# Expert rows in transposable stripes: VectorE in place of TensorE for turning the token rows

## The chip, the cores and the metric

One core of a Trainium2 chip runs the whole program. The metric is the device time of one execution in microseconds. TensorE (PE) multiplies, VectorE (DVE) and ScalarE (ACT) work elementwise, GpSimd (POOL) issues the indirect transfers, and SyncE (SP) issues the plain ones, in the order of its program: while it waits for a semaphore, nothing behind that wait is issued.

## The reference, cut to what matters

The input is 4 sequences of 3072 tokens with 256 features. A two-dimensional Fourier transform is taken (real part), each token then goes to one of 8 experts, and a channel mix follows.

```python
X = np.fft.fft(np.fft.fft(x, axis=1), axis=2).real
# expert stage, N = 12288 tokens, D = 256, F = 1024, 8 experts
expert_idx = np.argmax(logits, axis=1)
for e in range(E):
    mask = expert_idx == e
    h = np.maximum(x[mask] @ w1[e], 0.0)
    out[mask] = gate_w[mask, None] * (h @ w2[e])
# channel mix on out: two mixes with the previous token, relu^2, sigmoid
```

## The kernel before

The program has three stages. The Fourier stage (to about 209 us of the span) works through four batches; it leaves each batch's spectrum in `xr` (24 slots of 128 tokens), and GpSimd scatters these rows, sorted by expert, into the DRAM tensor `rows`. A row there is 256 features, the gate and the number of the row where the result belongs (`ROW` = 258 words, 1032 bytes). The expert stage (209 to 869 us) goes over `NB` = 55 blocks of `BT` = 256 rows, one block a step, each block of one expert only. The channel mix follows.

One step i of the expert stage, `m_step(i, s)` on each engine, with the buffer number s = i % 2:

- PE: `up` (48 matmuls of the first product, into four PSUM banks), `rows_in(i + 1)` (the next block's rows, four 128x128 transposes into PSUM bank 6), `down` (48 matmuls of the second product, in two halves j of 128 tokens).
- ACT: `hidden_a` four times (relu of a bank, the high part of `ht`), between them `w_high_part` (the next block's weights, high parts), `rows_a` (the high part of the next block's rows, `xgt`, from PSUM bank 6), and two `result` (gate times result, into `yo`).
- DVE: `hidden_v` four times (low part of `ht`), between them `w_low_part`, then `meta` (gates and row numbers out of `xg` into `gates` and `ids`), `rows_v` (low part of `xgt`), and two more `w_low_part`. In steps 0 to 5 it also finishes the gates and the block tables of the last batch.
- POOL: after each step's result, `scatter`: two indirect transfers of `yo` to the DRAM tensor `moe`, by `ids`. Ahead of the first of these stands the rest of the scatter of batch 2, in steps 4 to 7 stand six transfers each of batch 3, and in steps 12 to 14 one `w_split` subtraction each for the channel mix.
- SP: in `m_step(i)` it waits until block i's weights are split (`w_low`), issues `load_w(i + 2)` (2 MB, 128 pieces of 16 KB), waits for `m_meta` of step i (the buffer `xg[s]` is free then) and issues `load_rows(i + 2)` (one transfer of 258 KB, 128 pieces of 2064 bytes). Ahead of step 9 stand eight transfers of the padding rows (`load_tails`), ahead of step 10 three loads of the channel mix's weights. Each `load_w` and `load_rows` first reads its expert or its row number from SBUF (`value_load`).

All orders are written out by hand; every engine runs in program order. PE's `down(i)` waits for the four `hidden_v` of step i one after the other, its `up(i + 1)` for `rows_v`.

Of the kernel before, what the change touches and what calls it, by code (L numbers as in the profile page):

```python
# [28 lines left out]
P = 128  # L29
B, S, D = 4, 3072, 256  # L30
N2 = 24
J = 4
G = P // J
KP = N2 * J
NK = N2 // 2 + 1
# [42 lines left out]

C_ORDER = [0, 128] + list(range(2, 128, 2)) + list(range(1, 128, 2))
ORDER = C_ORDER + [D - c for c in C_ORDER[2:]]  # L80


def constants():
# [49 lines left out]
def fft_moe_channel_mix(nc, x, emb, tau, w_e, mu_k, mu_r, w_k, w_v, w_r, tab, out, rows, moe):  # L133
    ctx = ExitStack()
    with ctx:
        def sb(name, shape, dt=F32):
            return ctx.enter_context(nc.sbuf_tensor(name, shape, dt))[:]

        def sem(name):
            return ctx.enter_context(nc.semaphore(name))  # L140
# [43 lines left out]
        gates = [sb(f"gates{i}", [P, HB]) for i in range(2)]  # L184
        ids = [sb(f"ids{i}", [P, HB], I32) for i in range(2)]


        base = -(-nc.sbuf_base // 32) * 32
# [39 lines left out]
        yo_at = at[0]  # L228
# [14 lines left out]
        ht = part("ht", [2, FC, BT], F32R)  # L243
        assert at[0] <= xg_at
        at[0] = xg_at
        xg = [part(f"xg{n}", [HB, ROW]) for n in range(2)]
# [75 lines left out]
        m_meta = sem("m_meta")  # L322
        s_pad = sem("s_pad")
        s_half = sem("s_half")
        gathered = [sem(f"gathered{n}") for n in range(2)]
        m_xtr = sem("m_xtr")
        m_xt = sem("m_xt")
        m_up = sem("m_up")
        m_xh = sem("m_xh")
# [73 lines left out]
        def _(sp):  # L403
# [10 lines left out]
            def load_rows(i, s):  # L414

                r = sp.value_load(row_of[0:1, bass.ds(i, 1)], min_val=0, max_val=E * CAPR)
                sp.dma_start(xg[s].rearrange("p j c -> p (j c)"),
                             rows[bass.ds(r, BT), :].rearrange("(p j) c -> p (j c)", j=HB)).then_inc(gathered[s], 16)

            sp.dma_start(f1[:], tab["c_f1"]).then_inc(s_tab, 16)  # L420
            sp.dma_start(emb_in[0:E, :], emb).then_inc(s_emb, 16)
# [49 lines left out]
            def m_step(i, s):  # L471
                if i + 2 < NB:
                    sp.wait_ge(w_low, (i + 1) * WP)
                    load_w(i + 2, s)
                    sp.wait_ge(m_meta, i + 1)
                    load_rows(i + 2, s)

            for i in range(NB):
# [48 lines left out]
        def _(pe):  # L527
# [42 lines left out]
                    ins = mm(o, a(i), b_(k), start=first_ and n == 0, stop=last_ and n == 2)  # L570
                return ins

            def rows_in(i, s):
                pe.wait_ge(gathered[s], 16 * (i // 2 + 1))
                wait(pe, m_xt, i)
                for c in range(DC):
                    for j in range(HB):
                        last = tp(ps[:, 6, c * BT + j * P:c * BT + (j + 1) * P], xg[s][:, j, c * P:(c + 1) * P], ident[:])  # L578
                last.then_inc(m_xtr, 1)

            for b in range(B):

                for c in range(NC):
# [50 lines left out]
                for st in range(NK + 1):  # L634
                    if st < NK:
                        feature_dft(st)
                    if 0 <= st - 1 < NK:
                        sequence_dft(st - 1)
                    if b == B - 1 and st == NK - 2:
                        rows_in(0, 0)  # L640


            for n in range(2):
# [29 lines left out]

            def m_step(i, s):
                up(i, s)
                if not isinstance(i, int) or i + 1 < NB:
                    rows_in(i + 1, 1 - s)
# [76 lines left out]
        def _(act):  # L754
# [16 lines left out]
                copy(tot.rearrange("p h c -> p (h c)"), ps[0:TH * E, 7, 0:2 * P]).then_inc(d_totc, 1)  # L771

            def rows_a(i):
                act.wait_ge(m_xtr, i + 1)
                copy(xgt[:, 0, :, :].rearrange("p c t -> p (c t)"), ps[:, 6, :]).then_inc(m_xh, 1)

            def squares(b, k2):

# [49 lines left out]
            def result(i, s, j):  # L828
                act.wait_ge(m_down, i * HB + (j + 1))
                if j == 0:  # L830
                    act.wait_ge(m_meta, i + 1)
                    wait(act, scattered[s], i // 2 * (16 * HB))
                ins = nc.scalar.activation(yo[s][:, j, :], ps[:, 4 + j, 0:D], ACT.Copy,  # L833
                                           scale=gates[s][:, j:j + 1])
                ins.then_inc(m_y, 1)

            def m_step(i, s):
# [81 lines left out]
        def _(dve):  # L919
# [67 lines left out]
            def gate(b):  # L987
                link = chain(r_step, (b + 1) * R_STEPS + R_EXP)
                dve.wait_ge(r_exp, b + 1 + PRIME)
                link(v.tensor_reduce(gsum, ex, AX.X, ALU.add))  # L990
                link(v.tensor_scalar(gsum, gsum, 1e-9, None, ALU.add))
                link(v.reciprocal(gsum[:], gsum[:]))
                assert link.n[0] == R_STEPS - R_EXP
                xo = xr[XB[b]]
                copy(xo[:, 0:1, D:D + 1], gsum[:, 0:1].unsqueeze(2))
                copy(xo[:, 1:NK, D:D + 1], gsum[:, 1::2].unsqueeze(2))
                copy(xo[:, NK:N2, D:D + 1], gsum[:, N2 - 2:0:-2].unsqueeze(2))
                v.tensor_scalar(xo[:, :, D + 1:ROW], idc[:].unsqueeze(2), float(b * RB), None, ALU.add  # L998
                                ).then_inc(gate_done, 1)

            def place(b):
# [69 lines left out]
            def w_low_part(i, s, q):  # L1071
# [2 lines left out]
                v.tensor_tensor(we[s][:, 1, c0:c0 + WQ], we_raw[s][:, c0:c0 + WQ],  # L1074
                                we[s][:, 0, c0:c0 + WQ].bitcast(F32), ALU.subtract).then_inc(w_low, 1)

            def rows_v(i, s):
                dve.wait_ge(m_xh, i + 1)
                v.tensor_tensor(xgt[:, 1, :, :].rearrange("p c t -> p (c t)"), ps[:, 6, :],
                                xgt[:, 0, :, :].rearrange("p c t -> p (c t)").bitcast(F32), ALU.subtract).then_inc(m_xt, 1)  # L1080

            for b in range(B):
                xo = xr[XB[b]]
# [15 lines left out]
                for st in range(NK + 1):  # L1099
# [25 lines left out]
                        tier_b(False)  # L1125
                    if b == 2 and st == 10:
                        tier_c(False)
                    if b == B - 1 and st == NK - 1:
# [6 lines left out]
            def meta(i, s):  # L1135
                dve.wait_ge(gathered[s], 16 * (i // 2 + 1))
                wait(dve, m_y, i * HB - HB)
                wait(dve, scattered[s], i // 2 * (16 * HB))
                copy(gates[s][:], xg[s][:, :, D:D + 1].rearrange("p j o -> p (j o)"))
                copy(ids[s][:], xg[s][:, :, D + 1:ROW].rearrange("p j o -> p (j o)")).then_inc(m_meta, 1)  # L1140

            def hidden_v(i, n):
                dve.wait_ge(m_hh, i * (FC // 2) + (n + 1))
# [3 lines left out]

            def m_step(i, s):
                more = not isinstance(i, int) or i + 1 < NB
                hidden_v(i, 0)  # L1150
                if more:
                    w_low_part(i + 1, 1 - s, 0)
                hidden_v(i, 1)
                if more:
                    w_low_part(i + 1, 1 - s, 1)
                hidden_v(i, 2)
                hidden_v(i, 3)
                meta(i, s)
# [73 lines left out]
        def _(pool):  # L1232
# [10 lines left out]
            g.memset(tailc[:, :, D + 1:ROW], FAR).then_inc(d_init, 1)  # L1243
# [20 lines left out]
            moe_flat = moe.rearrange("b r c -> (b r) c")  # L1264

            def scatter(i, s):
                pool.wait_ge(m_meta, i + 1)
                for j in range(HB):
                    pool.wait_ge(m_y, i * HB + (j + 1))
                    g.indirect_dma_start(out=moe_flat, in_=yo[s][:, j, :], in_offset=None,  # L1270
                                         out_offset=bass.IndirectOffsetOnAxis(ap=ids[s][:, j:j + 1], axis=0),
                                         bounds_check=last_result, oob_is_err=False).then_inc(scattered[s], 16)

            for i in range(NB):
# [41 lines left out]
```

## Time and profile before

| what | us |
|---|---|
| runs, median of 3 (lowest, highest) | 1517.86 (1515.67, 1519.12) |
| the profiled execution | 1520.16 |
| its span, first to last instruction | 1518.4 |
| PE busy | 1470.5 (97%) |
| DVE busy | 1006.2 (66%) |
| ACT busy | 884.3 (58%) |
| POOL busy | 250.5 (17%) |
| mean granted TensorE clock | 0.986 |

The rows below come from the profile page and from queries of the same trace. Times are from the start of the span. In a timeline row, the bracket tells how long the engine had been idle and who released it. A busy share is a mean over stages; what a step costs is read from the chain that sets its end.

### The profile page before, as it was taken

Reading aid. Unit: us, or ns where it says so; the run is one execution under the profiler, and the core shown is the slowest. Engines: PE = TensorE matmul, PEld = TensorE weight load, DVE = VectorE, ACT = ScalarE, POOL = GpSimd, SP = SyncE. Lnnn points to the kernel's source line nnn. Section 1 sums busy time; section 2 is a strip of 40 time slices with the busy share of each in tenths; the row PEclk is TensorE's granted clock in tenths of the full one; section 3 lists DMA queues with packets and bytes.
Section 4 is the critical chain, followed back from the end, with each engine's and each line's share of the span. In section 5 each row is a group of like instructions: output and inputs, shape, how many; then the busy total and the mean of one; then the engine's idle time right before and its main releaser. Section 6 shows DMA issues by size and latency. Waiting matters only on the chain.

```text
span 1518.4 us, 29616 instructions
## 1 busy us (share of the span) xinstructions
PE 1470.5 (97%) x10894; PEld 1403.0 (92%) x10894; DVE 1006.2 (66%) x1765; ACT 884.3 (58%) x1706; POOL 250.5 (17%) x225
## 2 busy tenths in 40 slices
PE   6998889999999999999999879999999999999998
PEld 6887789999999999999999878999999998999998
DVE  4767776866666666666666456767576767667673
ACT  1654475666656666566665455656565656556563
POOL 2146436722311111111111100000000000000000
PEclk8999999999999999999999979999999999999999
DMA  8225366887656665666556111110111101010100
GB/s 245 67 76 156 107 215 236 292 291 275 216 214 233 224 213 208 212 230 231 211 208 214 64 42 56 29 55 28 52 31 32 51 28 55 28 55 28 55 14 28
DMA packets 64339, 201.47 MB, mean 133 GB/s; under 512 B 14246, under 2 KB 40725, under 8 KB 55576
## 3 DMA queue, kind: packets, MB, share of 16 engines
q1 hardware_dynamic: 54392, 175.42, 34.4%
q0 software_dynamic: 9888, 25.28, 4.5%
q8 instruction: 34, 0.56, 0.2%
q14 instruction: 25, 0.20, 0.0%
HBM read 160.44 MB, written 42.06 MB: 133 GB/s over the span
## 4 chain that ended last, share of the span: by engine, by line
PE 91%; DVE 3%; DMA 2%; ACT 1%; issue 1%; SPq 1%; POOL 1%; POOLq 0%; DVEq 0%; ACTq 0%
PE ps L570 78%; PE ps L596 4%; PE ps L630 3%; PE ps L697 1%; PE ps L578 1%; PE ps L619 1%; PE ps L620 1%; DMA we_raw<-w_e 1%; POOL rows L1252 1%; DVE we L1074 0%; SPq L486 0%; DMA tau_b<-tau 0%; DVE k2f L1209 0%; DMA moe<-yo,ids 0%; DVE k_split L1202 0%
## 5 line engine op out<-in xcount | busy, mean ns | idle before, releaser
L570 PE MATMUL ps<-we,ht 128*128 128x256 f32 x2640 | 330.5, 284 | 1.6 <-DVE ht L1144 1.6
L570 PE MATMUL ps<-xgt,we 128*128 128x256 f32 x2640 | 322.9, 282 | 4.6 <-DVE we L1074 3.8
L570 PEld LDWEIGHTS ps<-xgt,we 128*128 128x128 f32 x2640 | 317.5, 189 | 5.3 <-issue 4.2
L570 PEld LDWEIGHTS ps<-we,ht 128*128 128x128 f32 x2640 | 319.8, 188 | 2.5 <-DVE ht L1144 2.2
L570 PE MATMUL ps<-w_split,k_split 128*128 128x256 f32 x2304 | 280.5, 283 | 0.1
L570 PEld LDWEIGHTS ps<-w_split,k_split 128*128 128x128 f32 x2304 | 278.2, 192 | 0.3 <-DVE k_split L1202 0.3
L1074 DVE TENSOR_TENSOR we<-we_raw,we 128x1024 fp32r<-128x1024 f32 x220 | 263.3, 1217 | 16.7 <-ACT we L767 16.7
L1144 DVE SCALAR_TENSOR_TENSOR ht<-ps,ht 128x512 fp32r<-128x512 f32 x220 | 146.2, 684 | 192.3 <-ACT ht L825 192.2
L570 PE MATMUL ps<-x_split,w_split 128*128 128x512 f32 x1152 | 268.7, 393 | 4.4 <-DVE x_split L1196 4.4
L570 PEld LDWEIGHTS ps<-x_split,w_split 128*128 128x128 f32 x1152 | 216.7, 190 | 49.1 <-DVE x_split L1196 4.8
L897 ACT ACTIVATE relu<-ps 128x512 f32<-128x512 f32 x192 | 115.0, 599 | 205.2 <-PE ps L570 205.2
L767 ACT CAST we<-we_raw 128x1024 fp32r<-128x1024 f32 x220 | 226.0, 1055 | 3.5 <-DMA we_raw<-w_e 3.5
L825 ACT ACTIVATE ht<-ps 128x512 fp32r<-128x512 f32 x220 | 132.2, 602 | 99.0 <-PE ps L570 98.9
L1270 POOL DMA_INDIRECT moe<-yo,ids x110 | 111.3, 1012 | 448.5 <-ACT yo L833 443.1
L1209 DVE TENSOR_TENSOR k2f<-relu 128x512 f32<-128x512 f32 x192 | 132.9, 692 | 48.7 <-ACT relu L897 33.8
L833 ACT ACTIVATE yo<-ps,gates 128x256 f32<-128x256 f32 x110 | 52.1, 475 | 149.3 <-PE ps L570 144.4
L1202 DVE TENSOR_TENSOR k_split<-k2f,k_split 128x512 fp32r<-128x512 f32 x192 | 131.5, 685 | 2.1
L891 ACT CAST k_split<-k2f 128x512 fp32r<-128x512 f32 x192 | 117.8, 613 | 11.2 <-DVE k2f L1209 11.2
L1218 DVE TENSOR_TENSOR yc<-ps,sig 128x1024 f32<-128x1024 f32 x24 | 29.4, 1224 | 136.7 <-PE ps L570 136.7
L1252 POOL DMA_INDIRECT rows<-xr,pos x96 | 103.3, 1076 | 63.0 <-DVE xr L998 35.0
L1192 DVE SCALAR_TENSOR_TENSOR xmix<-xc,mu,tmix 128x512 f32<-128x512 f32 x96 | 67.9, 748 | 22.2 <-ACT tmix L879 22.2
L879 ACT ACTIVATE tmix<-xc,omm 128x512 f32<-128x512 f32 x96 | 64.2, 716 | 23.1 <-DVE xc L1186 20.2
(134 smaller groups left out, 1285.7 us busy)
## 6 DMA issues: line engine op xcount, KB each, us to landing
we_raw<-w_e SPq DMA_DIRECT2D x55, 2048.0 KB, 8.4
xg<-rows SPq DMA_DIRECT2D x55, 258.0 KB, 2.7
xin<-x SPq DMA_DIRECT2D x16, 768.0 KB, 5.8
xm<-moe SPq DMA_DIRECT2D x24, 512.0 KB, 3.9
out<-yc SPq DMA_DIRECT2D x24, 512.0 KB, 3.2
rows<-tailc SPq DMA_DIRECT2D x9, 258.0 KB, 2.9
moe<-yo,ids POOLq DMA_INDIRECT x110
f<-c_f SPq DMA_DIRECT2D x1, 1664.0 KB, 16.9
```

The lines of the kernel that those rows point to most:

```text
L570: ins = mm(o, a(i), b_(k), start=first_ and n == 0, stop=last_ and n == 2)
L767: copy(we[s][:, 0, c0:c0 + WQ], we_raw[s][:, c0:c0 + WQ]).then_inc(w_high, 1)
L825: nc.scalar.activation(ht[:, 0, 2 * n:2 * n + 2, :].rearrange("p f t -> p (f t)"), ps[:, n, :], ACT.Relu).then_inc(m_hh, 1)
L891: copy(k_split[:, 0, f, :], k2f[f % 2][:]).then_inc(c_kh, 1)
L897: nc.scalar.activation(relu[f % 2][:], ps[:, 2 + f % 2, :], ACT.Relu).then_inc(c_relu, 1)
L1074: v.tensor_tensor(we[s][:, 1, c0:c0 + WQ], we_raw[s][:, c0:c0 + WQ], we[s][:, 0, c0:c0 + WQ].bitcast(F32), ALU.subtract).then_inc(w_low, 1)
L1144: v.scalar_tensor_tensor(ht[:, 1, 2 * n:2 * n + 2, :].rearrange("p f t -> p (f t)"), ps[:, n, :], 0.0, ht[:, 0, 2 * n:2 * n + 2, :].rearra ...
L1192: v.scalar_tensor_tensor(xmix[:, m_, c, :], xc[s][:, c, 1:TC + 1], mu[:, m_, c:c + 1], tmix[:, m_, c, :], ALU.mult, ALU.add).then_inc(c_mi ...
L1202: v.tensor_tensor(k_split[:, 1, f, :], k2f[f % 2][:], k_split[:, 0, f, :].bitcast(F32), ALU.subtract).then_inc(c_kl, 1)
L1209: v.tensor_tensor(k2f[f % 2][:], relu[f % 2][:], relu[f % 2][:], ALU.mult).then_inc(c_k2, 1)
L1252: g.indirect_dma_start(out=rows, in_=xr[XB[b]][:, SLOTS[t], :], in_offset=None, out_offset=bass.IndirectOffsetOnAxis(ap=pos[:, b * N2 + t: ...
L1270: g.indirect_dma_start(out=moe_flat, in_=yo[s][:, j, :], in_offset=None, out_offset=bass.IndirectOffsetOnAxis(ap=ids[s][:, j:j + 1], axis= ...
```

## The change

The rows of a block no longer come as whole rows on 128 partitions, but as four stripes a = 0 to 3. Stripe a goes to partitions 32a to 32a + 31 and holds 64 features of all 256 tokens: partition 32a + i has, for each of 8 groups t of 32 tokens, features 64a to 64a + 63 of token 32t + i. In DRAM that is 256 pieces of 256 bytes a stripe, 1024 a block. One VectorE instruction (`rows_t`, 128x512) then transposes all 32x32 blocks into `xgf` in SBUF, which has the features on the partitions. TensorE's `rows_in` is gone. The order of the features on the partitions differs from before, so the first weight's rows are reordered on the host (`BLOCKS`). `rows_a` and `rows_v` read `xgf` and not PSUM.

Gate and row number come in a transfer of their own (`meta`, 256 pieces of 8 bytes), the row number as an integer, and ScalarE and GpSimd read them from there; VectorE's `meta` and its two small instructions are gone. The buffer `meta[s]` is free for block i only when the scatter of block i - 2 has landed, so SP waits for that scatter inside `load_rows`. The stripes' buffer is free as soon as `rows_t` has read it (`m_xf`).

```diff
             def load_rows(i, s):
                 r = sp.value_load(row_of[0:1, bass.ds(i, 1)], min_val=0, max_val=E * CAPR)
-                sp.dma_start(xg[s].rearrange("p j c -> p (j c)"),
-                             rows[bass.ds(r, BT), :].rearrange("(p j) c -> p (j c)", j=HB)).then_inc(gathered[s], 16)
+                for a in range(P // Q):
+                    sp.dma_start(xg[s][a * Q:(a + 1) * Q].rearrange("i t c f -> i t (c f)"),
+                                 rows[bass.ds(r, BT), a * DC * Q:(a + 1) * DC * Q].rearrange("(t i) f -> i t f", i=Q)
+                                 ).then_inc(gathered[s], 16)
+                if i >= 2:
+                    sp.wait_ge(scattered[s], (i - 2) // 2 * (16 * HB) + 16 * HB)
+                sp.dma_start(meta[s][:], rows[bass.ds(r, BT), D:ROW].rearrange("(j p) c -> p j c", j=HB)
+                             ).then_inc(meta_in[s], 16)
...
                     load_w(i + 2, s)
-                    sp.wait_ge(m_meta, i + 1)
+                    sp.wait_ge(m_xf, i + 1)
                     load_rows(i + 2, s)
...
-            def rows_in(i, s):
-                pe.wait_ge(gathered[s], 16 * (i // 2 + 1))
-                wait(pe, m_xt, i)
-                for c in range(DC):
-                    for j in range(HB):
-                        last = tp(ps[:, 6, c * BT + j * P:c * BT + (j + 1) * P], xg[s][:, j, c * P:(c + 1) * P], ident[:])
-                last.then_inc(m_xtr, 1)
...
             def rows_a(i):
-                act.wait_ge(m_xtr, i + 1)
-                copy(xgt[:, 0, :, :].rearrange("p c t -> p (c t)"), ps[:, 6, :]).then_inc(m_xh, 1)
+                act.wait_ge(m_xf, i + 1)
+                copy(xgt[:, 0, :, :], xgf[:]).then_inc(m_xh, 1)
...
+            def rows_t(i, s):
+                dve.wait_ge(gathered[s], 16 * (P // Q) * (i // 2 + 1))
+                wait(dve, m_xt, i)
+                v.transpose(xgf.rearrange("p c (t i) -> p c t i", i=Q), xg[s].rearrange("p t c f -> p c t f")
+                            ).then_inc(m_xf, 1)
...
             def m_step(i, s):
                 more = not isinstance(i, int) or i + 1 < NB
+                if more:
+                    rows_t(i + 1, 1 - s)
                 hidden_v(i, 0)
...
-                meta(i, s)
...
             def scatter(i, s):
-                pool.wait_ge(m_meta, i + 1)
+                pool.wait_ge(meta_in[s], 16 * (i // 2 + 1))
```

On SP the work around the loads of rows reads as follows in the program before; `we_raw_78` and `we_raw_79` are the two weight buffers, and this is the piece from the rows of block 2 to the weights of block 3:

```order
L416 TENSOR_LOAD row_of [waits m_meta]
L416 ISA x2
L417 ISA
L417 DMA xg_83<-rows 128x516
L411 TENSOR_LOAD expert_of [waits w_low]
L411 ISA x2
L412 ISA
L412 DMA we_raw_78<-w_e 128x4096
```

And the same place in the changed program, from the last stripe of block 2 to the first instruction for the rows of block 3:

```order
L421 DMA xg_83<-rows 32x8x64
L426 ISA [waits scattered0]
L426 DMA meta<-rows 128x2x2
L414 TENSOR_LOAD expert_of [waits w_low]
L414 ISA x2
L415 ISA
L415 DMA we_raw_78<-w_e 128x4096
L419 TENSOR_LOAD row_of [waits m_xf]
```

Between the rows of block 2 and the weights of block 3 there now stands a wait for the scatter of block 0 (`scattered0`); in general `load_w(i + 3)` stands behind the scatter of step i, which it did not before.

## Rows read from the trace of the kernel before

**Rows 1.** Chain of waits, 480 to 530 us: start, length, what.

```profile
483.69 0.44 PE ps L578 x4
484.13 11.43 PE ps L570 x96
```

**Rows 2.** Groups by line, VectorE: count, busy us, mean ns, idle before.

```profile
L1074 DVE TENSOR_TENSOR we<-we_raw,we 128x1024 fp32r<-128x1024 f32 x220 | 263.3, 1217 | 16.7 <-ACT we L767 16.7
...
L1202 DVE TENSOR_TENSOR k_split<-k2f,k_split 128x512 fp32r<-128x512 f32 x192 | 131.5, 685 | 2.1
```

**Rows 3.** Timeline of step 24, 501 to 514 us, all engines.

```profile
501.59 5.84 PE L570 MATMUL ps<-xgt,we 128*128 128x256 f32 x48
...
502.54 0.97 POOL L1270 DMA_INDIRECT moe<-yo,ids  x1 [1.28 <-ACT yo L833]
...
503.92 0.69 DVE L1144 SCALAR_TENSOR_TENSOR ht<-ps,ht 128x512 fp32r<-128x512 f32 x1 [3.76 <-ACT ht L825]
...
504.86 1.23 DVE L1074 TENSOR_TENSOR we<-we_raw,we 128x1024 fp32r<-128x1024 f32 x1 [0.25 <-ACT we L767]
...
507.74 1.28 DVE L1144 SCALAR_TENSOR_TENSOR ht<-ps,ht 128x512 fp32r<-128x512 f32 x2
...
509.67 2.35 DVE L1074 TENSOR_TENSOR we<-we_raw,we 128x1024 fp32r<-128x1024 f32 x2
...
512.76 0.33 SPq L412 DMA_DIRECT2D we_raw<-w_e  x1
```

**Rows 4.** Weight loads: the page's DMA issues, and the tile's time to landing.

```profile
we_raw<-w_e SPq DMA_DIRECT2D x55, 2048.0 KB, 8.4
...
DMA to landing us min/median/max: 7.7/8.4/12.5
```

**Rows 5.** DMA packets: 1019.2 to 1020.8 (1 KB), 1.75 to 2.05 (384 bytes), 871.4 to 871.8 us.

```profile
q1 hardware_dynamic: 477, 0.49, 100.5%
...
q1 hardware_dynamic: 94, 0.03, 48.9%
...
q0 software_dynamic: 48, 0.00, 7.7%
```

**Rows 6.** GpSimd's timeline, 223 to 248 us.

```profile
223.58 4.20 POOL L1260 TENSOR_TENSOR rinv<-sumsq,half 128x24 f32<-128x24 f32 x1 [21.12 <-ACT square L786]
...
245.09 0.97 POOL L1270 DMA_INDIRECT moe<-yo,ids  x1 [0.30 <-issue]
246.37 0.97 POOL L1270 DMA_INDIRECT moe<-yo,ids  x1 [0.30 <-issue]
```

**Rows 7.** Chain of waits, 200 to 400 us: start, length, what.

```profile
246.37 2.40 DMA moe<-yo,ids
...
249.84 5.94 PE ps L570 x48
...
337.53 12.53 DMA we_raw<-w_e
```

**Rows 8.** SP's timeline, 205 to 350 us: start, length of issue.

```profile
222.07 0.33 SPq L412 DMA_DIRECT2D we_raw<-w_e  x1
...
318.68 8.66 SPq L468 DMA_DIRECT2D rows<-tailc  x8
328.10 0.35 SPq L412 DMA_DIRECT2D we_raw<-w_e  x1
```

**Rows 9.** Timelines of PE (330 to 372 us) and of GpSimd (355 to 410 us).

```profile
333.09 5.84 PE L570 MATMUL ps<-xgt,we 128*128 128x256 f32 x48
...
359.19 5.84 PE L570 MATMUL ps<-xgt,we 128*128 128x256 f32 x48
...
371.05 1.11 PE L570 MATMUL ps<-xgt,we 128*128 128x256 f32 x8
...
374.45 1.86 POOL L1270 DMA_INDIRECT moe<-yo,ids  x1 [0.30 <-issue]
```

**Rows 10.** Busy time by windows; after the busy times the granted clock, DMA share, GB/s.

```profile
208.00:212.00 4.00, 2.40 (x11) 2.43 (x12) 3.72 (x4) 0.00 (x0) 0.00 (x0) 0.66 0.00 0
```

More of the change, by code:

```diff
@@ L32 @@
 J = 4
+Q = 32
 G = P // J
@@ L80 @@
 ORDER = C_ORDER + [D - c for c in C_ORDER[2:]]
+BLOCKS = np.arange(D).reshape(P // Q, D // P, Q).transpose(1, 0, 2).reshape(D)
 def constants():
@@ L183, in fft_moe_channel_mix @@
         row_of = sb("row_of", [1, NB], I32)
-        gates = [sb(f"gates{i}", [P, HB]) for i in range(2)]
-        ids = [sb(f"ids{i}", [P, HB], I32) for i in range(2)]
+        meta = [sb(f"meta{i}", [P, HB, 2]) for i in range(2)]
         base = -(-nc.sbuf_base // 32) * 32
@@ L227, in fft_moe_channel_mix @@
         emb_sq = part("emb_sq", [D])
-        yo_at = at[0]
+        yo_at = xg_at + 2 * HB * D + 3 * DC * BT
+        assert at[0] <= yo_at
         at[0] = yo_at + 2 * HB * D
@@ L245, in fft_moe_channel_mix @@
         at[0] = xg_at
-        xg = [part(f"xg{n}", [HB, ROW]) for n in range(2)]
+        xg = [part(f"xg{n}", [BT // Q, DC, Q]) for n in range(2)]
+        xgf = part("xgf", [DC, BT])
         xgt = part("xgt", [2, DC, BT], F32R)
@@ L321, in fft_moe_channel_mix @@
         w_in = [sem(f"w_in{n}") for n in range(2)]
-        m_meta = sem("m_meta")
         s_pad = sem("s_pad")
@@ L325, in fft_moe_channel_mix @@
         gathered = [sem(f"gathered{n}") for n in range(2)]
-        m_xtr = sem("m_xtr")
+        m_xf = sem("m_xf")
+        meta_in = [sem(f"meta_in{n}") for n in range(2)]
         m_xt = sem("m_xt")
@@ L638, in _ @@
                         sequence_dft(st - 1)
-                    if b == B - 1 and st == NK - 2:
-                        rows_in(0, 0)
             for n in range(2):
@@ L675, in m_step @@
                 up(i, s)
-                if not isinstance(i, int) or i + 1 < NB:
-                    rows_in(i + 1, 1 - s)
                 if isinstance(i, int) and i == 1:
@@ L830, in result @@
                 if j == 0:
-                    act.wait_ge(m_meta, i + 1)
+                    act.wait_ge(meta_in[s], 16 * (i // 2 + 1))
                     wait(act, scattered[s], i // 2 * (16 * HB))
                 ins = nc.scalar.activation(yo[s][:, j, :], ps[:, 4 + j, 0:D], ACT.Copy,
-                                           scale=gates[s][:, j:j + 1])
+                                           scale=meta[s][:, j, 0:1])
                 ins.then_inc(m_y, 1)
@@ L997, in gate @@
                 copy(xo[:, NK:N2, D:D + 1], gsum[:, N2 - 2:0:-2].unsqueeze(2))
-                v.tensor_scalar(xo[:, :, D + 1:ROW], idc[:].unsqueeze(2), float(b * RB), None, ALU.add
+                v.tensor_scalar(xo[:, :, D + 1:ROW].bitcast(I32), idc[:].unsqueeze(2), float(b * RB), None, ALU.add
                                 ).then_inc(gate_done, 1)
@@ L1075, in w_low_part @@
                                 we[s][:, 0, c0:c0 + WQ].bitcast(F32), ALU.subtract).then_inc(w_low, 1)
+            def rows_t(i, s):
[3 more added lines that the diff above has]
+                            ).then_inc(m_xf, 1)
             def rows_v(i, s):
                 dve.wait_ge(m_xh, i + 1)
-                v.tensor_tensor(xgt[:, 1, :, :].rearrange("p c t -> p (c t)"), ps[:, 6, :],
-                                xgt[:, 0, :, :].rearrange("p c t -> p (c t)").bitcast(F32), ALU.subtract).then_inc(m_xt, 1)
+                v.tensor_tensor(xgt[:, 1, :, :], xgf[:], xgt[:, 0, :, :].bitcast(F32), ALU.subtract).then_inc(m_xt, 1)
             for b in range(B):
@@ L1127, in _ @@
                         tier_c(False)
+                    if b == B - 1 and st == NK - 2:
+                        rows_t(0, 0)
                     if b == B - 1 and st == NK - 1:
@@ L1133, in _ @@
                 w_low_part(0, 0, q)
[L1135 to L1140, printed above, removed]
             def hidden_v(i, n):
@@ L1242, in _ @@
             pool.wait_ge(d_init, 1)
-            g.memset(tailc[:, :, D + 1:ROW], FAR).then_inc(d_init, 1)
+            g.memset(tailc[:, :, D + 1:ROW].bitcast(I32), int(FAR)).then_inc(d_init, 1)
             last_row, last_result = pool.to_reg(E * CAPR - 1), pool.to_reg(NROWS - 1)
@@ L1270, in scatter @@
                     g.indirect_dma_start(out=moe_flat, in_=yo[s][:, j, :], in_offset=None,
-                                         out_offset=bass.IndirectOffsetOnAxis(ap=ids[s][:, j:j + 1], axis=0),
+                                         out_offset=bass.IndirectOffsetOnAxis(ap=meta[s][:, j, 1:2].bitcast(I32), axis=0),
                                          bounds_check=last_result, oob_is_err=False).then_inc(scattered[s], 16)
@@ L1306 @@
         "w_e": c(np.concatenate([
-            moe_w1[:, ORDER, :].reshape(E, DC, P, F).transpose(0, 2, 1, 3).reshape(E, P, DC * F),
+            moe_w1[:, ORDER, :][:, BLOCKS, :].reshape(E, DC, P, F).transpose(0, 2, 1, 3).reshape(E, P, DC * F),
             moe_w2.reshape(E, FC, P, D).transpose(0, 2, 1, 3).reshape(E, P, FC * D)], 2)), "mu_k": c(moe2_mu_k.reshape(DC, P).T), "mu_r": c(moe2_mu_r.reshape(DC, P).T),
```

## The prediction, made before the changed kernel ran

> **What bounds the kernel now.** I read the chain of waits first. In the middle of the expert stage it is TensorE and nothing else: 11.43 us of products and 0.44 us of transposes in turn [rows 1], so a step of 11.87 us. The timeline of one step then tells how much room the others have. Counted from the start U of a step's `up` (501.59), VectorE begins its first low part at +2.33 after 3.76 us of idling, once more stands still for 0.25 us, and has its fourth low part done at 509.02, +7.43 [rows 3]. TensorE is ahead of nobody by much there, so what delays VectorE by more than about half a microsecond reaches TensorE. Last I read who issues the loads, and when. SP issues the weights of the block after next at 512.76, 0.74 us after the last low part of the weights (509.67 + 2.35) [rows 3]; that is 0.7 us before the next step begins. They land after 8.4 us in the median, 7.7 at the least [rows 4], against 13.9 us until ScalarE wants them. This lead of some 5.5 us is what the change spends.
>
> **What it removes.** The four transposes on TensorE, 0.44 us a step [rows 1]; there are 55 of them, 24.2 us, all on the chain. That is the whole gain there can be. VectorE's two small instructions went beside other work: nothing.
>
> **What it adds on VectorE.** One 128x512 instruction, `rows_t`. The trace has no such transpose. From below and as my value: the 512-column instruction out of SBUF, 0.69 us; from above, two passes, the 1024-column row, 1.22 us [rows 2]. It stands ahead of the first `hidden_v`, where VectorE idles for 3.76 us [rows 3]. As long as the stripes are there 0.7 us before +2.33 it costs nothing. If they come later, it holds all four low parts behind it. ScalarE's and VectorE's reads of `xgf` in place of PSUM: nothing, the wait is elsewhere.
>
> **What it adds in transfers.** 1024 pieces of 256 bytes for 128 of 2064. A piece's price: share times 16 engines times window by packets, so 1.005 x 16 x 1.6 / 477 = 54 ns for 1 KB, 0.489 x 16 x 0.3 / 94 = 25 ns for 384 bytes, and 0.077 x 16 x 0.4 / 48 = 10 ns for the smallest [rows 5]. 256 bytes lie between the last two, nearer to 25: I take 20 ns, 1024 x 20 / 16 = 1.3 us a block; the ends are 0.7 us and, should a piece cost as much as one of 1 KB, 3.5 us. The stripes are queued behind the weights, so this comes on top of the weights' landing. The Trainium skill, page "DMA: Bandwidth & Descriptors", first table, speaks against the change here: below 512 B a transfer is said to be done as read-modify-write. The 384-byte row does not show a jump (25 ns is under half of 54). By that rule, read as a doubled price, the stripes would take 2.6 us.
>
> **What it adds as a wait.** This is the dear part. SP now waits for the scatter of step i before it loads `meta` for block i + 2, and behind that wait are queued `load_w(i + 3)` and the stripes of block i + 3. In time from U of step i + 1, which is the end of step i: the second scatter is issued at 502.54, +0.95 [rows 3]; it lands 2.40 us later where no weight load is under way [rows 7]; `meta` is issued in some 0.4 us (0.33 for the instruction and a register or two); the expert's number is read and the weights issued 0.74 us on, together +4.5. In the kernel before this was -0.7. The weights land 8.0 us later (between 7.7 and 8.4, since one of two scatters no longer meets them), the stripes 1.3 us behind: +13.8 after the end of step i. They are wanted at the head of step i + 2, two steps on. From there to the end of that step: `rows_t` 0.69, from the first low part's start to the fourth one's end 5.10 less 0.25 of idling = 4.85 [rows 3], then 30 of the 96 products are left, 30 x 11.43 / 96 = 3.57, and 0.1 for the signal, together 9.2 us. So two steps together last at least 13.8 + 9.2 = 23.0, a step 11.5 us. TensorE alone would need 11.43. **I take 11.55** for the ordinary step: a gain of 0.32 and not of 0.44 us.
>
> **Where the hold is longer.** (a) *Step 2.* GpSimd is far behind here: after a `rinv` that waits 21.12 us for ScalarE (223.58) it has the rest of batch 2 to scatter, and the two scatters of step 0 are issued only at 245.09 and 246.37 [rows 6]. Nothing in the change makes this earlier. The second lands at 248.77 [rows 7]. Before, the weights of block 3 were issued at 222.07 [rows 8]; now at 248.77 + 0.4 + 0.74 = 249.9. They land at 258.2 (8.0, and 0.3 for the scatters of step 1 beside them), the stripes at 259.5. In step 2 ScalarE stands before `w_high_part(3)` and VectorE before `rows_t(3)`, and TensorE's `down(2)` gets no input from about 240 on. Its end is 259.5 + 9.2 = 268.7. The clock comes on top: where TensorE had idled ahead of the expert stage, the granted clock of 208 to 212 us was 0.66, so part of that stretch at 1.2 instead of 2.4 GHz [rows 10]; I add 1.5 us. Step 3 starts at 270.2 and not at 249.84 [rows 7]: **+20.4**. (b) *Steps 3 to 9*, with the rows of batch 3 on the DMA engines: weights 8.4 and 0.3 more give 11.85 a step, 83.0 against 333.09 - 249.84 = 83.25: **-0.3**. (c) *Steps 10 and 11.* The eight tails take SP 9.4 us (318.68 less 0.7 for reading the row number, to 327.34) [rows 8], and these now begin only after the scatter of step 8 and its `meta`, 0.95 + 2.40 + 0.4 = 3.75 into step 9. The weights of block 11 go out at 3.75 + 9.4 + 0.74 = 13.9, the stripes are in at 23.2, step 10 ends at 32.4 and, with 11.8 for step 9, lasts 20.6. The weights of block 12 landed 350.06 - 328.10 = 22.0 us after the issue of block 11's [rows 7, 8]; with one more block of stripes 23.3 and their own 1.3, then 9.2: step 11 lasts 14.0 by the same count. With 1 us for the clock 35.6, against 359.19 - 333.09 = 26.1 [rows 9]: **+9.5**. (d) *Steps 12 to 16.* GpSimd's `w_split` makes the second scatter start at 374.45, 3.4 after the end of the step (371.05) [rows 9] and not 0.95: three times 2.45 us later, half of it a step, (23.0 + 2.45) / 2 = 12.7 for four steps, 11.5 for one: **+3**. (e) *Steps 17 to 53*, 37 of them at 11.55: **-12**.
>
> **The sum.** 20.4 - 0.3 + 9.5 + 3 - 12 = +20.6 us on the profiled execution's 1520.2, 1540.8. The median of the runs lies 2.3 us below the profiled execution: 1538.5, **about 1539 us**. The gain of 24.2 us is in it, as the steps are compared whole. In the Fourier stage one transposing instruction on VectorE takes the place of four on TensorE: nothing.
>
> **Rivals.** *The stripes are late in every step.* If a piece costs as much as 1 KB (3.5 us a block) and `rows_t` two passes, two steps last 23.0 + 2.15 + 0.53 = 25.7, a step 12.85: (e) becomes +36, (b) +9, and the others 13 more, +88, 1606 us. Halfway, stripes of 2.6 us give 12.15 a step: (e) +10, (b) +4, in all some +48, 1566. The sentence on transfers below 512 B would lead here. For it: 256 bytes is a size the trace does not have, and the two steps' sum has only 0.15 us to spare. Against it: the 384-byte row. *The hold is free except in step 2, and the kernel is faster.* Mechanism: SP's wait uses up a lead that nobody needed. If weights and stripes land within 13.2 us of a step's end, each of the steps 3 to 53 gets its 0.44 back, also those of (c) and (d) because the lead there is taken up by two steps and not one: 52 x 0.44 = 22.9 against 18 for step 2, -5, 1513 us. It decides at a cost of (a), (c) and (d) together of under 21 us; by the rows of GpSimd and SP, (a) is that much alone. *The stall of step 2 does not come*: that would need GpSimd's scatter of step 0 some 10 us before 245.09, and 12 transfers of batch 2 stand ahead of it. I see no way.
>
> **How the numbers follow.** Forecast 0.6, between 1525 (least ends: step 2 at 18.5, ordinary step 11.43, steps 10 and 11 at +7, in all +7) and 1552. Late stripes 0.27, 1552 to 1606. Faster 0.08. In between, within 0.2%, 0.05. A measurement of this kernel can tell about 0.2%, 3 us. The range that leaves out 2 in 10 goes from 1520 to 1582. Faster 0.08, same 0.05, slower 0.87.
>
> **What would show it.** In the changed profile: the four transposes gone from the chain; TensorE idle for 15 us or more in step 2, released by VectorE, with the chain going back through `rows_t`, the stripes and `load_w` to the scatter of step 0; weights issued at +4.5 and not -0.7 in the ordinary step; steps of 11.43 to 11.7 us there, perhaps long and short in turn; step 10 near 20 us. I am wrong if `load_w(3)` is issued before 245 us, if `rows_t` takes over 1.3 us, or if stripes land over 2.5 us behind the weights.

## The result, and the profile after

The changed kernel is slower: 1553.7 us in the median of four runs (1551.55 to 1558.85) against 1518.0 us (1515.67 to 1519.12), a ratio of 1.023 with a 95% interval of 1.0205 to 1.0255. That is +35.7 us where +20.6 was forecast. The time lies inside the range of 1520 to 1582 us, but 15 us above the forecast of 1539, and 2 us above 1552, where the forecast's own part ended and that of late stripes began; which of the two it is, the number alone doesn't tell. The profiled execution is the slowest of the four, 1558.85 us with a span of 1557.0, so the comparison of traces below has +38.6 us to explain.

The page of the changed kernel: the busy times, the shares of the chain that ended last, and two groups (count, busy us, mean ns, idle before).

```profile
PE 1466.2 (94%) x10674; PEld 1388.7 (89%) x10674; DVE 1032.1 (66%) x1710; ACT 887.8 (57%) x1706; POOL 256.0 (16%) x225
...
PE 67%; DMA 12%; DVE 7%; SPq 5%; issue 5%; ACT 2%; POOL 2%; DVEq 0%; POOLq 0%; ACTq 0%
...
L1071 DVE TENSOR_TENSOR we<-we_raw,we 128x1024 fp32r<-128x1024 f32 x220 | 266.1, 1232 | 1.9 <-ACT we L764 1.8
...
L1077 DVE STREAM_TRANSPOSE xgf<-xg 128x512 f32<-128x512 f32 x55 | 39.1, 712 | 216.7 <-DMA xg<-rows 216.4
```

TensorE has 220 matmuls fewer and is busy 4.3 us less (the 24 us of [rows 1] are gone from the chain, but the matmuls around the new stops ran at a lower clock: the mean granted clock is 0.974 and was 0.986). The chain before was TensorE nearly alone in the expert stage. Now DMA, SP's queue, "issue" and VectorE stand in it with 29% together. VectorE waits 216.4 us for the stripes in front of `rows_t`, in 50 waits of 4.3 us in the mean: the stripes are what comes last.

The waits of the changed kernel by cause (us in total, times, longest):

```profile
DVE xgf L1077 <- DMA xg<-rows: 216.4, 50, 26.1
...
PE ps L579 <- DVE ht L1141: 44.4, 32, 19.5
...
ACT we L764 <- DMA we_raw<-w_e: 39.0, 9, 21.8
```

And the wait that the change put into SP's program (SP's own waits, same form):

```profile
SPq L426 <- DMA moe<-yo,meta: 411.4, 51, 33.4
```

One of TensorE's waits is 19.5 us long. It is step 2, and the chain of 228 to 275 us (start, length, what) tells how it comes about, the counterpart of [rows 6] and [rows 7]:

```profile
246.09 0.97 POOL moe L1268
247.06 0.30 issue
247.37 2.41 DMA moe<-yo,meta
249.94 0.40 SPq L426
...
251.11 0.36 SPq L415
...
253.50 0.47 SPq L421
254.15 6.21 DMA xg<-rows
260.39 0.71 DVE xgf L1077
261.10 0.58 DVE ht L1141
...
265.20 6.00 PE ps L579 x36
```

GpSimd issues the second scatter of step 0 at 247.37. It lands, SP loads `meta` (L426), then the weights of block 3 (L415, at 251.11 where 222.07 was their time before, [rows 8]), then the four stripes (L421). At 260.39 `rows_t` runs, and step 2 ends at 271.0.

The same chain in an ordinary step, 568 to 591 us:

```profile
569.19 2.41 DMA moe<-yo,meta
571.76 0.39 SPq L426
...
572.92 0.36 SPq L415
...
575.87 6.60 DMA xg<-rows
582.50 0.08 DVE xgf L1077
...
587.30 4.59 PE ps L579 x36
```

Step 25 ends at 568.24 and the weights leave at 572.92, +4.68 (before: -0.7). The stripes behind them are what `rows_t` of step 27 waits for until 582.5, and from there the chain runs on to the end of step 27 at 591.7, where it starts again.

Steps by the starts of `up` (us; steps 0 and 1 differ by 0.8 us in all, the Fourier stage and the mix by 0.7):

| steps | before | after | difference | forecast |
|---|---|---|---|---|
| 2, to the start of step 3 (249.84 before, 271.02 after) | 14.6 | 36.0 | +21.2 | +20.4 |
| 3 to 9 | 83.2 | 89.5 | +6.2 | -0.3 |
| 10 and 11 | 26.1 | 35.0 | +8.9 | +9.5 |
| 12 to 16 | 59.3 | 67.3 | +8.0 | +3 |
| 17 to 53 | 439.1 | 433.3 | -5.7 | -12 |
| an ordinary step of these | 11.87 | 11.71 | -0.16 | -0.32 |

The difference of step 2 is that of the start of step 3, as the prediction counted it.

### The profile page after: what moved, and what is told of

Its sections match the earlier page's. It is cut to its first block, busy times and chain, and to the rows that moved or that the text cites. A ratio compares the mean times of both kernels' runs of the same rounds, so it can differ in the third digit from the quotient of the medians.

```text
span 1557.0 us, 29654 instructions
## 1 busy us (share of the span) xinstructions
PE 1466.2 (94%) x10674; PEld 1388.7 (89%) x10674; DVE 1032.1 (66%) x1710; ACT 887.8 (57%) x1706; POOL 256.0 (16%) x225
## 4 chain that ended last, share of the span: by engine, by line
PE 67%; DMA 12%; DVE 7%; SPq 5%; issue 5%; ACT 2%; POOL 2%; DVEq 0%; POOLq 0%; ACTq 0%
PE ps L579 56%; DMA xg<-rows 7%; PE ps L597 4%; DMA moe<-yo,meta 3%; PE ps L631 3%; DVE we L1071 2%; DVE ht L1141 2%; SPq L421 2%; PE ps L694 1%; PE ps L620 1%; PE ps L621 1%; DMA we_raw<-w_e 1%; POOL rows L1250 1%; SPq L426 1%; SPq L414 1%
## 5 line engine op out<-in xcount | busy, mean ns | idle before, releaser
L579 PE MATMUL ps<-we,ht 128*128 128x256 f32 x2640 | 344.5, 287 | 45.3 <-DVE ht L1141 44.4
L579 PEld LDWEIGHTS ps<-we,ht 128*128 128x128 f32 x2640 | 329.2, 192 | 56.2 <-issue 32.7
L1268 POOL DMA_INDIRECT moe<-yo,meta x110 | 116.2, 1057 | 478.5 <-ACT yo L830 475.3
L1077 DVE STREAM_TRANSPOSE xgf<-xg 128x512 f32<-128x512 f32 x55 | 39.1, 712 | 216.7 <-DMA xg<-rows 216.4
L830 ACT ACTIVATE yo<-ps,meta 128x256 f32<-128x256 f32 x110 | 52.3, 476 | 155.7 <-PE ps L579 154.4
```

## The experiments

The theory is H, the hold: SP's wait for the scatter of step i ahead of `load_w(i + 3)` and the stripes makes the kernel slower, the rest of the change is good for the 0.44 us a step of [rows 1]. The rivals: S, the small pieces and VectorE's transposing cost by themselves; and, as a question of its own, where the 15 us of the miss lie. The kernels of this part ran later than the result above, in three groups, the first and third on chip 0 and the second on chip 6 (for the result above the record names none); a ratio compares a kernel with the kernel before in the same group, on the same chip. In all three groups every kernel, the one before included, takes some 50 us more, all of it outside the ordinary steps (the last section). Medians of the kernel before: 1571.4, 1569.8 and 1577.3 us.

**The hold alone**, in the kernel before:

```diff
                     load_rows(i + 2, s)
+                    sp.wait_ge(scattered[s], i // 2 * (16 * HB) + 16 * HB)
```

> The kernel before with one wait more: SP waits for the scatter of step i ahead of load_w(i + 3), as the changed kernel does; no stripes, transposes on TensorE. Theory H: step 2 about 18 us longer, step 10 about 6, a few us around w_split, ordinary step 11.87 us unchanged since the weights still land ahead of +2.3 us: 1543 to 1548 us. Rival S: 1517 to 1522 us, as the wait alone would be hidden.

1593.5 us, ratio 1.0132 (1.0081 to 1.0182). Step 2 takes 34.9 us and step 10 21.8 us, as in the changed kernel; the ordinary step stays at 11.867. By the ratio that is 1538 us where the kernel before takes 1518, somewhat less than the 1543 to 1548 expected: in these groups step 2 of the kernel before is itself longer (21.7 us in `before_again`), so the hold adds only 13.2 us there. The waits of step 2 (276 to 312 us) in this kernel:

```profile
ACT we L768 <- DMA we_raw<-w_e: 19.7, 1, 19.7
...
PE ps L579 <- DMA xg<-rows: 16.7, 1, 16.7
```

One added line, no stripes and no `rows_t`, and TensorE stands still for 16.7 us. In the ordinary step the weights leave at +4.1 instead of -0.7, and that costs nothing here, as the chain of 640 to 680 us shows:

```profile
644.29 0.44 PE ps L579 x4
644.73 11.43 PE ps L571 x96
656.15 0.44 PE ps L579 x4
```

**The hold taken away** from the changed kernel: four buffers for `meta`, so that SP waits for the scatter of block i - 4, which has long landed. ScalarE's loop takes four steps a turn, so that the buffer's number is known.

```diff
-meta = [sb(f"meta{i}", [P, HB, 2]) for i in range(2)]
+meta = [sb(f"meta{i}", [P, HB, 2]) for i in range(4)]
...
-                if i >= 2:
-                    sp.wait_ge(scattered[s], (i - 2) // 2 * (16 * HB) + 16 * HB)
+                if i >= 4:
+                    sp.wait_ge(scattered[s], (i - 4) // 2 * (16 * HB) + 16 * HB)
```

> The changed kernel with four buffers for gates and row numbers, so that SP waits for the scatter of block i - 4 and not of block i - 2 ahead of the weights; stripes, transposes on VectorE and all orders stay. Theory H (the time is lost by SP's hold ahead of load_w): the whole loss goes and the 0.44 us a step come through, ordinary step 11.43 us, step 2 near 12 to 14 us, weights issued at -0.7 us again, 1494 to 1500 us. Rival S (the small pieces or the transposing instruction cost the time themselves): at least 1518 us, up to 1550.

1551.9 us, ratio 0.9873 (0.983 to 0.9915), faster than the kernel before. The chain of 600 to 650 us is one line:

```profile
599.95 50.13 PE ps L579 x420
```

The ordinary step is 11.453 us, TensorE alone, with the same 1024 pieces and the same `rows_t`. So S falls: stripes and `rows_t` cost nothing as long as they are there in time. In step 2 21.5 us remain against 14.6 in the kernel before at first, but 21.7 in `before_again` in these groups.

The two runs together also show that the parts of the change don't simply add up. Alone the hold costs 1.3%; between `meta4` and the changed kernel it costs 3.8% (0.9873 against 1.0248). Without stripes the ordinary step has room for weights that leave 4.8 us later, with them it hasn't.

A second time, beside a profile of the kernel before on the same chip:

> The version with four buffers for gates and row numbers once more, timed in five rounds: ordinary step 11.45 us, ratio to before 0.982 to 0.989, so 15 to 25 us faster.

> The kernel before, for its trace on this chip. If the chip of the earlier experiments is used again: the expert stage begins near 250 us instead of 210, in stops without a releaser on every engine, and its ordinary step is 11.87 us all the same.

`meta4_again` has 0.9923 (0.9897 to 0.9949) over 12 runs, less gain than expected, though still faster. The ordinary step is again 11.453. In the profiled execution steps 5 and 7 last 20.0 and 19.4 us (17.3 and 13.9 in `before_again`, whose one time is 1580.3 us), by stops that the last section tells of. The two ratios' intervals overlap between 0.9897 and 0.9915.

**The hold moved by one block**: `meta` of block i + 1 is loaded behind the stripes of block i + 2.

```diff
                     load_rows(i + 2, s)
+                if i >= 1 and i + 1 < NB:
+                    load_meta(i + 1, 1 - s)
```

> The changed kernel with two buffers, but SP loads the gates of block i + 1 behind the weights and stripes of block i + 2, one step later. Theory H: free wherever the scatter lands in time; only the weights of block 4 stand behind the late scatter of step 0, so step 3 lasts some 20 us and the rest is as with four buffers: 1503 to 1509 us. Rival S: 1518 us or more.

1565.7 us, ratio 0.9957 (0.9932 to 0.9982). Step 2 is down to 13.1 us, and step 3 takes 24.6: the same late scatter is met one block later. Behind the tails the hold is still felt, step 10 takes 17.9 us (11.9 in `meta4`). The ordinary step is 11.453. Expected was somewhat more gain in all (0.990 to 0.994, as a ratio).

**Buffers of their own for blocks 2 and 3**, the hold as it is from block 4 on:

```diff
-                if i >= 2:
+                if i >= 4:
                     sp.wait_ge(scattered[s], (i - 2) // 2 * (16 * HB) + 16 * HB)
```

> The changed kernel with buffers of their own for the gates of blocks 2 and 3, nothing else. Theory H: the 20 us of step 2 go (some 2 to 4 us come back in steps 3 and 4), the rest of the hold stays: 1534 to 1538 us. Rival S: no change, 1552 to 1556 us.

1588.1 us, ratio 1.0128 (1.0061 to 1.0196); the four runs lie in two pairs, 1577.6 and 1580.6, 1595.6 and 1597.1, and the profile is of the fastest. Step 2 takes 13.1 us and not 34.9, steps 12 to 16 and the ordinary step (11.722) are those of the changed kernel. Of the 21.8 us of step 2 some 7.6 come back in steps 3 to 9 (97.6 against 90.0 in `after_again`).

**The changed kernel itself**, in the second group, for the ratios:

> The changed kernel once more, beside the others of this call and before on the same chip. In the first four experiments all kernels, before too, lost some 40 us more in the Fourier stage and the first steps, in stops that the profile gives no releaser for; so ratios count there. Theory H: ratio to before 1.020 to 1.026, or on a chip with those stops 1.015 to 1.025, as part of step 2's hold then falls beside them; step 2 over 30 us, step 10 over 20 us.

1607.3 us, ratio 1.0248 (1.0203 to 1.0292): the result holds here. Step 2 takes 34.9 us, step 10 22.4, the ordinary step 11.78.

**The transposes of TensorE alone**: the kernel before with three of its four `tp` left out from block 1 on.

```diff
-                for c in range(DC):
-                    for j in range(HB):
+                for c in range(DC if full else 1):
+                    for j in range(HB if full else 1):
```

> The kernel before with one of the four transposes of each step (three left out, so most of the rows are not computed on; block 0 keeps all four). It measures the gain that there is to have: 3 x 0.11 = 0.33 us in 54 steps, 17.8 us less than before, ratio 0.987 to 0.990; the ordinary step 11.54 us. A theory in which the transposes are hidden would give 1.000.

1552.6 us, ratio 0.9894 (0.9856 to 0.9932), ordinary step 11.545. Three transposes are worth 11.867 - 11.545 = 0.32 us, so four are worth 0.43: the gain was sized right, it is all on the chain (655 to 678 us):

```profile
654.65 0.11 PE ps L579
654.76 11.43 PE ps L570 x96
```

**`rows_t` behind the fourth `hidden_v`**, so that late stripes hold up no low part:

```diff
-                if more:
-                    rows_t(i + 1, 1 - s)
                 hidden_v(i, 0)
...
                 hidden_v(i, 3)
+                if more:
+                    rows_t(i + 1, 1 - s)
```

> The changed kernel with rows_t behind the four hidden_v in VectorE's order instead of ahead of them; SP's hold stays as it is. Theory H in the form of the prediction (late stripes reach TensorE only because rows_t stands ahead of the low parts): ordinary step 11.43 to 11.5 instead of 11.71, steps 4 to 7 about 2 us shorter each, steps 14 and 16 shorter too, steps 2 and 10 only 1 us shorter since ScalarE still waits for the weights: 18 to 24 us below the changed kernel, ratio to before 1.007 to 1.012. If instead the transposing instruction or the small pieces cost by themselves: no change from the changed kernel.

1598.1 us, ratio 1.0179 (1.0141 to 1.0217): 9 us better than the changed kernel in the same group (18 to 24 were expected). The ordinary step is 11.648 and not 11.43 to 11.5. The waits of the whole run and the chain of 640 to 690 us:

```profile
ACT xgt L772 <- DVE xgf L1077: 104.8, 54, 2.4
DVE we L1071 <- ACT we L764: 86.1, 105, 22.1
```

```profile
638.50 8.22 DMA we_raw<-w_e
...
647.25 1.06 ACT we L764
...
651.22 0.70 DVE ht L1141
...
651.96 27.50 PE ps L579 x228
```

Now ScalarE stands for `xgf` in front of `rows_a`, its two `result` and with them the scatters come later (the second at +1.9, before +0.95), the weights leave at +5.6 instead of +4.7, and ScalarE waits for the weights. The stripes are out of the cycle, the cycle is not gone: it goes through scatter, SP and weights too.

**Half the stripes**: two of the four left out from block 2 on.

> The changed kernel with only two of the four stripes loaded from block 2 on (the other half of the features stays that of an earlier block, so the result is not the reference's); SP's hold stays. It shortens the cycle from one step's end over scatter, weights and stripes to the end of the step after the next by some 0.85 us. If two steps share one hold, the ordinary step goes down by half of that at most, from 11.71 to 11.45 to 11.5 us, where TensorE alone sets it. If the hold is paid in each step by itself it would fall by the whole 0.85 if it could, and if the stripes play no part it stays at 11.7.

One run, 1594.8 us, so no ratio is taken from it. The ordinary step goes to 11.500 (11.712 in the changed kernel, 11.777 in `after_again`), and TensorE is alone in the chain of 640 to 690 us. The stripes' 512 pieces less are 0.64 us of the 1.3, and from the issue of the weights to the start of `rows_t` it takes 8.76 us instead of 9.43. So the stripes are in the cycle. That two steps share one hold isn't shown by this run: TensorE's own 11.45 ends the gain at 0.26 to 0.32 us, whether half or all of the 0.67 would have come through. It is shown by the chain of the changed kernel, which goes through a scatter, weights and stripes once in two steps (568 to 591 us above).

**The tails one by one**, in `meta4`: one transfer in each of the steps 7 to 14 instead of eight ahead of step 9.

```diff
-                if i == C_SPLIT_AT[0] - 3:
-                    load_tails()
...
+                if 7 <= i < 7 + E:
+                    load_tails(i - 7, i - 6)
```

> Four buffers for gates and row numbers, and the eight tails not in one go ahead of step 9 but one behind the loads of each of steps 7 to 14. Theory H: the full 0.44 us a step, and the stalls of steps 10 and 11 of the kernel before (26.1 us instead of 23.7) mostly gone as well: ratio to before 0.981 to 0.985, 1490 to 1496 us on a chip where before takes 1518. Rival: it equals the four buffers alone, 0.987.

1558.0 us, ratio 0.9906 (0.987 to 0.9942). Steps 10 and 11 take 22.8 us, 3.2 less than in `meta4`, and the ordinary step 11.393. But the median is not lower than that of `meta4`, whose interval it overlaps; steps 3 to 9 have 92.3 us against 85.0. No gain is shown.

The best version is `meta4`, 0.9873 and 0.9923 in its two groups.

## Why the prediction was right, and where it was short

**The mechanism.** All that the prediction asked the changed profile to show is there: no transposes in the chain, TensorE idle for 19.5 us in step 2 with the chain going back through `rows_t`, stripes and weights to the scatter of step 0, the weights at +4.68 (forecast +4.5) in the ordinary step, step 10 at 21.3 us (forecast near 20). `before_hold` and `meta4` show that the hold is the cause, and not only its company. None of the three signs of being wrong came: `load_w(3)` is issued at 251.11, `rows_t` takes 0.71 us, and the stripes of the ordinary step are in 1.0 us behind the weights.

**Removed work**: 0.44 us a step, borne out by `before_1tp`.

**`rows_t`**: 711 ns in every ordinary step. The value taken, 0.69, was the lower bound, from another 512-column instruction of [rows 2]; it was 0.02 short.

**The pieces of 256 bytes.** 20 ns was the interpolation. In the changed kernel, the DMA view of 556.39 to 558.05 us, a block of stripes:

```profile
DMA packets 1141, 0.32 MB, mean 195 GB/s; under 512 B 1129, under 2 KB 1129, under 8 KB 1140
...
q1 hardware_dynamic: 1104, 0.28, 83.4%
```

0.834 x 16 x 1.66 / 1104 = 20.1 ns. The Trainium skill, page "DMA: Bandwidth & Descriptors", first table, has transfers below 512 B done as read-modify-write; the prediction had read that as a doubled price and a rival. The trace does not agree with the doubling: a piece of 256 bytes costs 20 ns, less than one of 384 bytes in [rows 5]. By the byte it is dearer all the same, 12.8 bytes a ns against 19 for 1 KB. With this row the rival of late stripes falls, though the measured time lies in its part of the range: the stripes are late by the hold, not by their price. Its sum was also added up wrongly in the text: its terms give +91, not +88, and with half of the 13 us for the other parts +53, not +48.

**(a) Step 2**, +21.2 against +20.4. The scatter was issued at 247.37 and not 246.37, 1.0 us; the expert stage had begun 0.6 later and GpSimd's `rinv` 0.8 (224.34 against 223.58). The rest was as counted, and the clock, for which 1.5 us had been added, is seen here. Busy times by windows of the changed kernel, the granted clock behind them (PE, PEld, DVE, ACT, POOL, then PEclk, DMA share, GB/s), in this order a stretch of step 14, one of step 16, the end of step 2 and a stretch of step 18:

```profile
425.00:435.40 10.40, 7.53 (x48) 7.06 (x49) 10.04 (x10) 7.07 (x10) 3.72 (x1) 0.84 0.70 227
452.00:462.80 10.80, 8.34 (x55) 7.66 (x54) 8.22 (x10) 4.55 (x7) 0.97 (x1) 0.84 0.68 220
261.00:271.00 10.00, 9.08 (x48) 8.52 (x49) 9.27 (x15) 4.63 (x8) 0.98 (x1) 0.63 0.48 166
480.00:486.00 6.00, 5.80 (x48) 5.59 (x48) 5.04 (x6) 3.48 (x5) 1.19 (x1) 1.00 0.96 347
```

After the long stop of step 2 the mean granted clock is 0.63 for 10 us, most of it at 1.2 GHz: from `rows_t` to the end of the step 10.6 us instead of 9.2.

**(b) Steps 3 to 9**, +6.2 against -0.3: *a term mis-sized*. The step was costed with the rows of batch 3 as a 0.3 us delay of the weights. In fact the first two of the three pieces of the cycle are longer here. Two steps as the sum of three pieces: from a step's start to the issue of the weights, from there to the start of `rows_t`, from there to the end of that step. In steps 4 to 8 the means are 6.29 + 11.31 + 9.23 = 26.8 us, a step 13.4, where the prediction had 4.5 + 10.0 + 9.2 = 23.7, a step 11.85. From the chain of 296 to 340 us:

```profile
296.11 3.33 DMA moe<-yo,meta
...
304.65 8.24 DMA xg<-rows
...
323.08 4.42 DMA moe<-yo,meta
...
332.00 7.00 DMA xg<-rows
```

A scatter of `yo` takes 3.3 and 4.4 us to land and not 2.40 [rows 7]. In these steps GpSimd issues six transfers of batch 3 ahead of it and a load of weights is under way; which of the two delays it wasn't taken apart. The six transfers had been named in the description of the kernel before; the prediction used the landing time of a stretch without them.

**(c) Steps 10 and 11**, +8.9 against +9.5. The eight tails took SP from 352.74 to 361.85, 9.1 us, forecast 9.4; step 10 lasted 21.3 and step 11 13.8 us, forecast 20.6 and 14.0, and 1 us for the clock.

**(d) Steps 12 to 16**, +8.0 against +3: *also mis-sized*. Steps 14 and 16 last 16.5 and 15.9 us, and the two pairs 13 + 14 and 15 + 16 28.2 and 27.3, forecast 25.45. By the same three pieces: 8.67 + 9.41 + 10.12 and 6.35 + 10.86 + 10.11. The last piece is 0.9 longer than 9.2, at a granted clock of 0.84 (above); the prediction had added nothing for the clock here. In the pair 13 + 14 the rest of the miss is in the first piece, costed at 4.5 + 2.45 = 6.95: the second scatter was issued at +3.8 and not +3.4, and took 3.53 us to land. Of its 1.1 us more than 2.40, 0.9 are the length of the instruction itself:

```profile
411.10 1.90 POOL L1268 DMA_INDIRECT moe<-yo,meta  x1 [0.30 <-issue]
```

The scatter of 2.40 us was one of 0.97. The row for this place had stood in [rows 9], with 1.86 us; the prediction took its start and not its length. In the pair 15 + 16 the first piece is shorter than costed, and the second is 1.5 longer: the weights land at 450.18, 8.35 us after their issue, but the stripes 2.5 us behind them.

```profile
444.82 7.84 DMA xg<-rows
```

Why these stripes took longer than the others stays open. At the head of this pair VectorE and GpSimd met. The timeline of the changed kernel, 428 to 438 us:

```profile
431.22 5.65 DVE L1071 TENSOR_TENSOR we<-we_raw,we 128x1024 fp32r<-128x1024 f32 x2
431.68 4.11 POOL L1281 TENSOR_TENSOR w_split<-w_raw,w_split 128x1536 fp32r<-128x1536 f32 x1 [7.93 <-ACT w_split L852]
...
435.94 1.80 POOL L1268 DMA_INDIRECT moe<-yo,meta  x1 [0.15 <-issue]
```

VectorE's two instructions, 2.35 us before ([rows 3]), take 5.65, the first 1.22 and the second, which began at 432.35, 4.52; `w_split` takes 4.11 and not 3.49. VectorE had stood 7.4 us for stripes, and so falls on `w_split`. This meeting is striking, but not where the miss comes from: TensorE does not stop behind it, and in `after_again`, which has the same slow instruction, the pair 15 + 16 lasts 23.6 us. The Trainium skill, page "GPSIMD Engine Reference", section "Architecture", says that GpSimd's SBUF port is shared with VectorE; the rows agree with that, and the last section tells what the other traces show of it. The prediction had not looked at what a shifted VectorE would meet.

**(e) Steps 17 to 53**, -5.7 against -12. The three pieces are 4.74 + 9.43 + 9.26 = 23.4 us for two steps, where 4.5 + 9.3 + 9.2 = 23.0 was the sum and 11.55 the value taken. Each of the three was sized right to 0.25 us, but their errors point the same way: 0.16 us a step, times 37, is the whole miss of 6 us. The first piece lacks 0.16 us between the landing and SP's instruction (571.60 to 571.76 in the chain), and in 6 of 35 cycles the weights left at +5.0 to +5.4; in two of these the second scatter was late. That the other two pieces fit so well is in part luck. From step 20 on the weights land after 8.47 us and not 8.0, the stripes 0.97 and not 1.3 behind them; from the start of `rows_t` to the last low part it takes 5.37 us and not 5.54, and then 3.9 are left and not 3.7 (36 matmuls in the chain, where 30 were counted). The forecast of a step as "half a cycle" is so close to TensorE's own 11.43 that a few tenths in the cycle take half the gain. A range of 11.43 to 11.9 for this term would have been fair.

**The rivals.** "The hold is free except in step 2, and the kernel is faster" fell by (c), (d) and (e): `meta_own23` has step 2 without its stall and is 1.0128. It was nearest in `meta_later`, where the hold is met a block later: the ordinary step is TensorE's alone there, and what is left of the hold stands in steps 3 and 10.

**Together**: 0.8 too little in (a), 6.5 in (b), 5.0 in (d), 6.3 in (e), 0.1 in the rest, and 0.6 too much in (c): the 18 us between +20.6 and +38.6. So the mechanism was right, and the terms mis-sized are the cycle with batch 3 beside it (b), the pairs behind `w_split` (d) and the ordinary step (e). By medians the miss is 15 us, as the profiled execution is 5 us above the median.

## What to carry to other kernels

A wait that is put into a queue of loads holds up everything behind it: cost it by the issue time of the next loads, not of its own transfer, and cost it again in each stretch where the resource that it waits for is late or shared. Two buffers more of 16 bytes a partition turned this change from +2.3% to -1%. Take the time from issue to landing from a row of that stretch, not from a quiet one: 2.40 us were 3.3 to 4.4 in one stretch and 3.53 in another. Where the new cycle is within a few tenths of the bound, its small constants decide the gain. And a change that is harmless by itself, as the hold in `before_hold`'s ordinary step and the stripes in `meta4`, can cost time together with another one that uses the same lead.

## What the runs showed of the hardware that was not expected

- Pieces of 256 bytes from HBM take 20 ns each on a DMA engine, against 25 for 384 bytes and 54 for 1 KB: by the piece small ones are cheap, by the byte they are dearer, and with the lead of `meta4` they cost nothing.
- A VectorE instruction on two SBUF operands, 1.22 us alone, took 4.50 to 4.53 us in all four traces in which it began while GpSimd's `w_split` ran (`after`, `after_again`, `meta_own23`, `stripes_half`), and ended 1.1 us behind it each time. The other way round, when such an instruction was under way as `w_split` began, it kept its 1.22 us and `w_split` was the longer one: with 0.76 us of it left 4.11 us and not 3.49 (`after`), with 0.95 left 4.30 (`before_hold`). So the one that began first made the other wait. Not with every operand: during `w_split` a low part that reads PSUM took its usual 0.69 us (`rows_t_later`, 448.06) and a transpose with one operand 0.71 (`meta4_tails`, 434.12). And not with every GpSimd instruction: the same kind of VectorE instruction took 1.23 us at 226.44 in the changed kernel, inside GpSimd's `rinv` of 4.20 us.
- A plain wait in the wrong queue costs time though it holds up no engine that computes: `before_hold` loses 1.3% by one line, while its ordinary step is the same to a nanosecond.
- In the three later groups, on two chips, the kernel before takes 1570 to 1577 us and not 1518. The ordinary step is 11.867 us in both traces; the expert stage starts at 253.7 and not 209.6 us. The waits up to there, of `before_again`, show stops that no work in the trace ends and that the same view of the first trace does not have:

```profile
ACT d L794 <- remote: 26.2, 4, 9.2
ACT eo L808 <- remote: 21.0, 4, 7.3
```

Steps 2, 5 and 7 are longer too (21.7, 17.3 and 13.9 us, where they were 14.6, 11.9 and 11.9). All of this stands in code that runs once and not in the loops. What the stops are was not tested, and it stays open; they blur the ratios of these groups, by which `meta4` lies anywhere between 0.983 and 0.995.
